# Logits moved into the bank of the turned SoLU row, and the expert picked ahead of the SoLU product

## The chip, the cores and the metric

The kernel runs on one core of one Trainium2 chip. The metric is the device time of one execution in microseconds (us), as the median of several runs. Matrix products run on TensorE, elementwise work and reductions on VectorE, activations and copies on ScalarE, small arithmetic and the scattered stores on GpSimd, and loads are issued by SyncE. A matrix product writes to PSUM, which has eight banks of 512 float32 columns for each of the 128 partitions.

## The reference

Three parts follow one another on 4608 tokens (8 batches of 576) of width 512.

- Attention through packed keys: for each batch and head, 32 pack rows attend to 576 keys and values (`p_packed`), and then the 576 queries attend to these 32 packed rows.
- A SoLU layer: `h = x @ w_in` (width 1024), `solu = h * softmax(h)`, a layer norm over the row with gains `g_ln`, and `ln @ w_out` (back to width 512).
- A mixture of 8 experts: `logits = x @ w_gate`, the expert of a token is the argmax, its weight the softmax probability of that expert, and the output is `gate * (relu(x @ w1[e]) @ w2[e])`.

## The kernel before

The tokens are cut into 36 tiles of 128 tokens, nine for each of four pairs of batches. After a setup, a pipelined loop over the tiles does attention, SoLU and the choice of the expert; each tile's rows are scattered to memory, sorted by expert. Then a second loop does the experts' two products for the sorted tiles. The change touches the first loop alone.

Every engine has a program of its own, written out by hand as a list of operations for one step t of the loop, and the engines meet only in semaphores. An engine executes its list in that order; when one operation waits, all that stands behind it on its engine waits too. Step t works on several tiles at once: scores and softmax of tile t+1, the up product (into the hidden row `h_ps`) and SoLU of tile t, the down product (into `y_ps`), gate logits and pick of tile t-1, and the rank of tile t-2 within its expert.

The loop's steps are of three kinds. Beside the work that every step has, 12 steps (here called **unit steps**, t mod 9 = 1, 3, 5, 7 in the first three pairs) compute the packed attention of one unit (two heads) of the next pair of batches, and 12 steps (**M steps**, t mod 9 = 2, 4, 6, 8 in the first three pairs) fold the packed rows of a unit into `w_in`, to give the matrix M of the next pair. The 12 others are **plain steps** (t = 0, 9, 18 and the nine tiles of the last pair). In three of the M steps (t = 8, 17, 26, **late M steps**) the scores of tile t+1 are computed after `up_hi` and not before it.

The lists of one step, in order, with the operations of unit and M steps in brackets:

- TensorE: `scores(t+1)`, [M: `k_turn_pp`], `rank(t-2)`, `up_hi(t)`, `up_lo(t)`, [unit: `k_scores`], `down_hi(t-1)` chunks 0 to 2 (six products), `logits_t(t-1)`, `down_hi` chunks 3 to 5, [M: `m_half` 0], `turn_logits(t-1)`, `down_hi` chunks 6 and 7, [unit: `k_turn`], `down_lo` 0 to 2, `turn_a(t+1)`, [M: `m_half` 1], [unit: `k_pack`], `down_lo` 3 to 7, `turn_z(t)`.
- VectorE: `max_s(t+1)`, `read_rank(t-2)`, [M: `k_lo`], `z_lo(t-1)`, `max_h(t)`, `sum_s(t+1)`, [unit: `k_max`], `solu(t)`, `row_sum(t)`, [M: `m_lo` 0], [unit: `k_sum`], `pick(t-1)`, `a_lo(t+1)`, [unit: `k_pp`], [M: `m_lo` 1].
- ScalarE: `z_hi(t-1)`, [M: `k_pt`], `exp_s(t+1)`, `z_raw(t-1)`, `exp_h(t)`, `copy_lt(t-1)`, [unit: `k_exp`], [M: `m_hi` 0], `squares(t)`, [unit: `k_et`], `a_hi(t+1)`, `exp_l(t-1)`, [M: `m_hi` 1], `copy_y(t-1)`. In the last pair one copy of expert weights a step (`first_hi`) comes ahead of `copy_y`.
- GpSimd: `factor(t-1)`, `probs(t+1)`, `place(t-2)`, `scatter_y(t-2)`.

Where these show in the profile: `turn_a` and `turn_z` share the helper line L1348 (they differ by what they read, `sbuf` and `hbuf`); `logits_t` is L1455, `turn_logits` L1461, `copy_lt` L732, `down_hi` L1428, `down_lo` L1435, `up_hi` L1407, `m_half` L1306, `m_hi` L650, `m_lo` L915, `k_max` L881, `k_turn` L1272, `k_et` L614 and L616, `k_pack` L1283, `solu` L1001, `squares` L715, `a_hi` L698 (L692 for the tiles of both batches), `z_raw` L727, `z_hi` L721. `pick` is six small VectorE operations, L1025 (reads the turned logits in PSUM) to L1039 (writes `hot`, the expert as a one-hot row). `sum_s` ends with L978. L487 is the first operation of `place`, which adds `hot` of the tile before to `hsum`; the last operation of `pick` waits for it.

Bank 7 holds the turned probabilities (`a_ps`, columns 0 to 255), the logits turned (`LT0`, 256) and turned back (`LG0`, 384), and the ranks (`RK0`, which shares 256). `turn_a(t+1)` writes this bank, so it waits until the first operation of `pick(t-1)` has read it. Banks 2 and 3 hold the turned SoLU row (`t_ps`): `turn_z` writes it, `z_hi` and `z_raw` read it, and then both banks lie idle until the next `turn_z`. The chain of a unit step is `k_scores` (TensorE), `k_max` (VectorE), `k_exp` (ScalarE), `k_turn` (TensorE), `k_et` (ScalarE), `k_pack` (TensorE). That of an M step is `m_half` (TensorE), `m_hi` (ScalarE), `m_lo` (VectorE) for each half; both halves use bank 6, so the second `m_half` waits for the `m_lo` of the first:

```python
                else:
                    pe.wait_ge(m_lo_done, 2 * u + h)
```

Of the kernel before, what the change touches and what calls it, by code (L numbers as in the profile page):

```python
# [17 lines left out]
ACT = mybir.ActivationFunctionType  # L18
AX = mybir.AxisListType

P = 128
B, H, S, DH, NPK = 8, 8, 576, 64, 32
D, F, E = H * DH, 1024, 8
# [21 lines left out]

LT0, LG0 = 2 * P, 3 * P
RK0 = LT0

ET0, KS0 = 2 * P, 512 - (S - 512)

# [1 line left out]
def wait(eng, sem, n):  # L54

    if not isinstance(n, int) or n > 0:
        eng.wait_ge(sem, n)


def moe_kernel(nc, q_t, k_t, v_t, p_t, w_moe, w_exp, g_ln, w_gate, out):  # L60
    y_dram = nc.dram_tensor("y_sorted", [E * CAP, YC], F32, kind="Internal").ap()
    ctx = ExitStack()
    with ctx:
# [55 lines left out]
        ident = sb("ident", [P, P], F32)  # L119
        mask_pp = sb("mask_pp", [P, P], F32)  # L120
        gln = sb("gln", [P, KF], F32)
        wog = sb("wog", [P, KF, NPK], F32)
# [12 lines left out]
        lg = sb("lg", [P, E], F32)  # L135
# [15 lines left out]
        lt = sb("lt", [P, P], F32)  # L151
# [4 lines left out]
        zraw = sb("zraw", [P, F], F32)  # L156
# [40 lines left out]
        a_ps = ps[:, 7, 0:2 * P]  # L197
        x_ps = ps[:, 6, :]
        g_ps = ps[:, 7, :]


        constants_set, zeroed, small_weights_in, numbers_set, numbers_cast, blanks_set = map(
# [66 lines left out]
        def there(t):  # L269
            return 0 <= t < NT  # L270
# [309 lines left out]
        def _(act):  # L580
# [142 lines left out]
            def z_raw(t):  # L723
                act.wait_ge(z_turned, t + 1)
                wait(act, logits_t_done, t)
                wait(act, z_lo_done, t)
                nc.scalar.activation(zraw[:].rearrange("p (a b) -> p a b", a=2), t_ps, ACT.Copy).then_inc(z_raw_done, 1)  # L727

            def copy_lt(t):
                act.wait_ge(logits_t_done, t + 1)  # L730
                wait(act, logits_turned, t)
                nc.scalar.activation(lt[:], g_ps[:, LT0:LT0 + P], ACT.Copy).then_inc(logits_copied, 1)  # L732

            def exp_l(t):
                q = t % 2
# [19 lines left out]
            for t in range(-1, NT + 1):  # L755
                u, v = unit_at(t), m_at(t)
                if there(t - 1):
                    z_hi(t - 1)
                if v is not None:
                    k_pt(v)  # L760
                if there(t + 1):
                    exp_s(t + 1)
                if there(t - 1):
                    z_raw(t - 1)
                if there(t):
                    exp_h(t)
                if there(t - 1):
                    copy_lt(t - 1)
                if u is not None:
                    k_exp(u)  # L770
                if v is not None:
                    m_hi(v, 0)
                if there(t):
                    squares(t)
                if u is not None:
                    k_et(u)
                if there(t + 1):
                    a_hi(t + 1)
                if there(t - 1):
                    exp_l(t - 1)  # L780
                if v is not None:
                    m_hi(v, 1)
                if LAST <= t < LAST + NCH:
                    first_hi(t - LAST)
                if there(t - 1):
                    copy_y(t - 1)
# [49 lines left out]
        def _(dve):  # L836
# [184 lines left out]
            def pick(t):  # L1021

                n = 4 * t
                dve.wait_ge(logits_turned, t + 1)
                nc.vector.tensor_reduce(lg[:], g_ps[:, LG0:LG0 + P].rearrange("p (k e) -> p e k", k=4)[:, 0:E, :],  # L1025
                                        AX.X, ALU.add).then_inc(pick_chain, 1)
                dve.wait_ge(pick_chain, n + 1)
                nc.vector.tensor_reduce(tok[:, 1:2], lg[:], AX.X, ALU.max).then_inc(pick_chain, 1)
                dve.wait_ge(pick_chain, n + 2)
                nc.vector.scalar_tensor_tensor(key[:], lg[:], tok[:, 1:2], rev[:],  # L1030
                                               ALU.is_equal, ALU.mult).then_inc(pick_chain, 1)
                wait(dve, logits_exp, t)
                nc.vector.tensor_scalar(lgs[:], lg[:], tok[:, 1:2], None, ALU.subtract).then_inc(logits_shifted, 1)
                dve.wait_ge(pick_chain, n + 3)
                nc.vector.tensor_reduce(tok[:, 2:3], key[:], AX.X, ALU.max).then_inc(pick_chain, 1)
                dve.wait_ge(pick_chain, n + 4)
                wait(dve, picked_summed, t)
                wait(dve, rank_summed, t)
                nc.vector.tensor_scalar(hot[:], key[:], tok[:, 2:3], None, ALU.is_equal).then_inc(picked, 1)  # L1039
# [10 lines left out]
            for t in range(-1, NT + 2):  # L1050
                u, v = unit_at(t), m_at(t)
                if there(t + 1):
                    max_s(t + 1)
                if there(t - 2):
                    read_rank(t - 2)
                if v is not None:
                    k_lo(v)
                if there(t - 1):
                    z_lo(t - 1)
                if there(t):  # L1060
                    max_h(t)
                if there(t + 1):
                    sum_s(t + 1)
                if u is not None:
                    k_max(u)
                if there(t):
                    solu(t)
                    row_sum(t)
                if v is not None:
                    m_lo(v, 0)  # L1070
                if u is not None:
                    k_sum(u)
                if there(t - 1):
                    pick(t - 1)
                if there(t + 1):
                    a_lo(t + 1)
                if u is not None:
                    k_pp(u)
                if v is not None:
                    m_lo(v, 1)  # L1080
# [128 lines left out]
        def _(pe):  # L1209
# [171 lines left out]
            def turn_a(t):  # L1381
                pe.wait_ge(probs_done, t + 1)
                if t == 0:
                    pe.wait_ge(m_lo_done, 2 * HP)
                if t >= 2:
                    pe.wait_ge(pick_chain, 4 * (t - 2) + 1)
                turn(a_ps, sbuf[:].rearrange("p a b -> p (a b)"), 2, probs_turned)

            def up_parts(t):
# [50 lines left out]
            def turn_z(t):  # L1440
                pe.wait_ge(solu_done, t + 1)
                wait(pe, z_raw_done, t)
                if t == 0:
                    pe.wait_ge(packed_lo, HP)
                    pe.wait_ge(keys_kept, HP)
                turn(t_ps, hbuf, KF, z_turned)

            def logits_t(t):
                pe.wait_ge(z_raw_done, t + 1)
                wait(pe, rank_read, t)  # L1450
                if t == 0:
                    pe.wait_ge(gates_chain, 6)
                for k in range(KF):
                    g = 32 * (k % 4)
                    mm = nc.tensor.matmul(g_ps[g:g + 32, LT0:LT0 + P], wog[:, k, :], zraw[:, k * P:(k + 1) * P],  # L1455
                                          start=(k < 4), stop=(k >= 4))
                mm.then_inc(logits_t_done, 1)

            def turn_logits(t):
                pe.wait_ge(logits_copied, t + 1)  # L1460
                nc.tensor.transpose(g_ps[:, LG0:LG0 + P], lt[:], ident[:]).then_inc(logits_turned, 1)  # L1461

            def rank(t):

# [6 lines left out]
            for t in range(-1, NT + 2):  # L1471
                u, v = unit_at(t), m_at(t)

                late = v is not None and (t + 1) % TPP == 0
                if there(t + 1) and not late:
                    scores(t + 1)
                if v is not None:
                    k_turn_pp(v)
                if there(t - 2):
                    rank(t - 2)  # L1480
                if there(t):
                    up_hi(t)
                if late:
                    scores(t + 1)
                if there(t):
                    up_lo(t)
                if u is not None:
                    k_scores(u, t)
                if there(t - 1):
                    down_hi(t - 1, range(0, 3))  # L1490
                    logits_t(t - 1)
                    down_hi(t - 1, range(3, 6))
                if v is not None:
                    m_half(v, 0)
                if there(t - 1):
                    turn_logits(t - 1)
                    down_hi(t - 1, range(6, KF))
                if u is not None:
                    k_turn(u)
                if there(t - 1):  # L1500
                    down_lo(t - 1, range(0, 3))
                if there(t + 1):
                    turn_a(t + 1)
                if v is not None:
                    m_half(v, 1)
                if u is not None:
                    k_pack(u)
                if there(t - 1):
                    down_lo(t - 1, range(3, KF))
                if there(t):  # L1510
                    turn_z(t)
# [112 lines left out]
```

## Time and profile before

| what | value |
|---|---|
| median of 3 runs | 1098.95 us (1098.42 to 1099.76) |
| the profiled execution | 1097.72 us, of which the span of the trace is 1096.1 us |
| TensorE busy with products | 1012.6 us, 92% of the span |
| VectorE, ScalarE, GpSimd busy | 505.2, 447.8, 284.9 us |
| mean granted TensorE clock | 0.966 of full speed |
| the first loop | from about 78 to 587 us of the span |

A product's record runs from its start to its modelled end, and the next starts before that end; so the distance between starts tells the cost better than the duration. In the timeline neighbouring instructions of one line are merged: the time is that of the first start, the second figure the time they cover, xN how many. A bracket names the idle time ahead of an instruction on its engine and what ended it.

### The profile page before, as it was taken

Reading aid. Unit: us, or ns where it says so; the run is one execution under the profiler, and the core shown is the slowest. Engines: PE = TensorE matmul, PEld = TensorE weight load, DVE = VectorE, ACT = ScalarE, POOL = GpSimd, SP = SyncE. Lnnn points to the kernel's source line nnn. Section 1 sums busy time; section 2 is a strip of 40 time slices with the busy share of each in tenths; the row PEclk is TensorE's granted clock in tenths of the full one; section 3 lists DMA queues with packets and bytes.
Section 4 is the critical chain, followed back from the end, with each engine's and each line's share of the span. In section 5 each row is a group of like instructions: output and inputs, shape, how many; then the busy total and the mean of one; then the engine's idle time right before and its main releaser. Section 6 shows DMA issues by size and latency. Waiting matters only on the chain.

```text
span 1096.1 us, 20129 instructions
## 1 busy us (share of the span) xinstructions
PE 1012.6 (92%) x5707; PEld 795.5 (73%) x5708; DVE 505.2 (46%) x1219; ACT 447.8 (41%) x767; POOL 284.9 (26%) x637
## 2 busy tenths in 40 slices
PE   7548999999999999999994999999999999999994
PEld 4336777777777777777873788888888888888883
DVE  3344666565666656576565252521152431234211
ACT  2344555555555555566552241421241322233110
POOL 1421222222222222245562121221121221222211
PEclk9758999999999999999997999999999999999998
DMA  9301222322122221151103551511152331111110
GB/s 354 108 11 51 67 66 78 97 87 88 58 61 85 87 79 38 37 195 50 39 20 116 193 191 48 190 40 48 38 170 69 114 125 38 46 40 38 48 38 29
DMA packets 64759, 92.62 MB, mean 84 GB/s; under 512 B 42944, under 2 KB 45120, under 8 KB 64704
## 3 DMA queue, kind: packets, MB, share of 16 engines
q1 hardware_dynamic: 55584, 61.96, 17.8%
q0 software_dynamic: 9120, 29.97, 8.0%
q8 instruction: 29, 0.48, 0.2%
q14 instruction: 26, 0.21, 0.1%
HBM read 70.37 MB, written 21.54 MB: 84 GB/s over the span
## 4 chain that ended last, share of the span: by engine, by line
PE 89%; DVE 3%; issue 2%; ACT 2%; DMA 1%; POOL 1%; SPq 0%; ACTq 0%; POOLq 0%; DVEq 0%
PE ps L1341 39%; PE ps L1428 12%; PE ps L1348 8%; PE ps L1407 7%; PE ps L1435 6%; PE ps L1416 3%; PE ps L1377 3%; PE ps L1306 2%; PE ps L1455 2%; PE ps L1263 2%; PE ps L1283 2%; DVE m_odd L915 1%; PE ps L1272 1%; PE ps L1219 1%; POOL w_in L440 1%
## 5 line engine op out<-in xcount | busy, mean ns | idle before, releaser
L1341 PE MATMUL ps<-W,xr 128*128 (+1 forms) x912 | 224.4, 401 | 2.4 <-DVE xr L1084 2.4
L1341 PE MATMUL ps<-W,zr 128*128 x912 | 222.2, 398 | 2.6 <-DVE zr L1157 2.6
L1341 PEld LDWEIGHTS ps<-W,xr 128*128 128x128 f32 x912 | 170.0, 190 | 41.7 <-DVE xr L1084 1.8
L1341 PEld LDWEIGHTS ps<-W,zr 128*128 128x128 f32 x912 | 168.3, 188 | 41.0 <-issue 2.8
L1428 PE MATMUL ps<-w_out,zr 128*128 128x512 f32 x576 | 156.8, 410 | 1.1 <-ACT zr L721 1.1
L1428 PEld LDWEIGHTS ps<-w_out,zr 128*128 128x128 f32 x576 | 101.9, 188 | 39.5 <-issue 16.9
L802 ACT ACTIVATE zr<-ps 128x1024 fp32r<-128x1024 f32 x38 | 39.0, 1025 | 196.6 <-PE ps L1348 196.6
L457 POOL TENSOR_TENSOR small<-half 128x1 f32<-128x1 f32 x77 | 21.6, 280 | 345.1 <-DVE yb L1169 195.4
L461 POOL TENSOR_TENSOR sbuf<-sbuf,msum 128x256 f32<-128x256 f32 x36 | 22.2, 616 | 283.0 <-DVE msum L978 283.0
L797 ACT ACTIVATE hbuf<-ps 128x1024 f32<-128x1024 f32 x38 | 38.8, 1022 | 137.6 <-PE ps L1341 137.6
L1084 DVE TENSOR_TENSOR xr<-ps,xr 128x512 fp32r<-128x512 f32 x39 | 26.9, 691 | 145.6 <-ACT xr L792 145.6
L1169 DVE TENSOR_SCALAR yb<-ps,gate 128x512 f32<-128x512 f32 x38 | 28.5, 751 | 137.7 <-PE ps L1341 137.7
L1435 PE MATMUL ps<-w_out,zr 128*128 128x512 f32 x288 | 81.4, 406 | 0.0
L708 ACT ACTIVATE hbuf<-ps,small 128x1024 f32<-128x1024 f32 x36 | 40.2, 1116 | 99.0 <-DVE small L996 99.0
L1348 PE MATMUL ps<-ident,hbuf 128*128 128x128 f32 x592 | 77.6, 275 | 1.0 <-ACT hbuf L797 0.7
L1348 PEld LDWEIGHTS ps<-ident,hbuf 128*128 128x128 f32 x592 | 69.8, 142 | 11.6 <-ACT hbuf L797 0.9
L1157 DVE TENSOR_TENSOR zr<-ps,zr 128x1024 fp32r<-128x1024 f32 x38 | 46.5, 1225 | 38.5 <-ACT zr L802 38.5
L1019 DVE TENSOR_TENSOR zr<-zraw,zr 128x1024 fp32r<-128x1024 f32 x36 | 44.1, 1225 | 36.4 <-ACT zraw L727 36.4
L1435 PEld LDWEIGHTS ps<-w_out,zr 128*128 128x128 f32 x288 | 51.6, 188 | 11.9 <-issue 2.1
L715 ACT ACTIVATE junk<-hbuf,small 128x1024 bf16<-128x1024 f32 x36 | 41.4, 1149 | 20.6 <-DVE small L1006 20.4
L1001 DVE SCALAR_TENSOR_TENSOR hbuf<-ps,hbuf 128x1024 f32<-128x1024 f32 x36 | 44.0, 1221 | 12.6 <-ACT hbuf L708 12.6
L996 DVE TENSOR_REDUCE small<-ps 128x1 f32<-128x1024 f32 x36 | 43.9, 1219 | 12.8 <-PE ps L1416 12.7
(216 smaller groups left out, 1486.5 us busy)
## 6 DMA issues: line engine op xcount, KB each, us to landing
raw_e<-w_exp SPq DMA_DIRECT2D x48, 512.0 KB, 5.0
qb<-y_sorted POOLq DMA_DIRECT2D x40, 257.0 KB, 3.0
vb<-v_t SPq DMA_DIRECT2D x16, 640.0 KB, 5.6
kb<-k_t SPq DMA_DIRECT2D x16, 576.0 KB, 4.4
qb<-q_t SPq DMA_DIRECT2D x144, 64.0 KB, 3.0
y_sorted<-pad SPq DMA_DIRECT2D x8, 257.0 KB, 4.2
raw_out<-w_moe SPq DMA_DIRECT2D x4, 512.0 KB, 5.0
raw_in<-w_moe SPq DMA_DIRECT2D x4, 512.0 KB, 14.3
```

Source lines behind the costliest of these rows:

```text
L708: nc.scalar.activation(hbuf[:].rearrange("p (a b) -> p a b", a=2), h_ps, ACT.Exp, bias=small[:, 0:1], scale=1.0, accum_out=small[:, 12 + q ...
L715: nc.scalar.activation(junk[:], hbuf[:], ACT.Square, bias=small[:, 16 + q:17 + q], scale=1.0, accum_out=small[:, 4 + q:5 + q]).then_inc(sq ...
L802: nc.scalar.activation(zr[:, 0, :].rearrange("p (a b) -> p a b", a=2), t_ps, ACT.Copy).then_inc(e_hidden_hi, 1)
L996: nc.vector.tensor_reduce(small[:, 0:1], h_ps, AX.XY, ALU.max, negate=True).then_inc(minus_max, 1)
L1001: nc.vector.scalar_tensor_tensor(hbuf[:].rearrange("p (a b) -> p a b", a=2), h_ps, 1.0, hbuf[:].rearrange("p (a b) -> p a b", a=2), ALU.mu ...
L1019: nc.vector.tensor_tensor(zr[:, 1, :], zraw[:], zr[:, 0, :].bitcast(F32), ALU.subtract).then_inc(z_lo_done, 1)
L1157: nc.vector.tensor_tensor(zr[:, 1, :].rearrange("p (a b) -> p a b", a=2), t_ps, zr[:, 0, :].bitcast(F32).rearrange("p (a b) -> p a b", a=2 ...
L1341: mm = nc.tensor.matmul(dst, lhs[:, a, k * P:(k + 1) * P], rhs(b, cols), start=(first and n == 0), stop=(last and n == 2))
L1348: mm = nc.tensor.transpose(dst[:, k * P:(k + 1) * P] if chunks <= 4 else dst[:, k // 4, (k % 4) * P:(k % 4 + 1) * P], src[:, k * P:(k + 1) ...
L1407: nc.tensor.matmul(h_ps[:, h, :], lhs[:, 0, :], M[i % 2][:, part, chunk, h * 512:(h + 1) * 512], start=(n == 0 and part == 0), stop=False)
L1428: nc.tensor.matmul(y_ps, zr[:, 0, k * P:(k + 1) * P], w_out[:, part, k * D:(k + 1) * D], start=(k == 0 and part == 0), stop=False)
L1435: mm = nc.tensor.matmul(y_ps, zr[:, 1, k * P:(k + 1) * P], w_out[:, 0, k * D:(k + 1) * D], start=False, stop=(k == KF - 1))
```

## The change

The logits, turned and turned back, move from bank 7 to bank 2, columns 0 to 255, so `turn_a` no longer waits for `pick`. In its place `turn_z(t)` waits for the first operation of `pick(t-1)`, and `logits_t` drops its wait for the rank. Four operations move: `logits_t` on TensorE ahead of the first six `down_hi` products, `turn_logits` ahead of the second six and of `m_half` 0, `copy_lt` on ScalarE ahead of `exp_h`, and `pick` on VectorE from behind `m_lo` 0 and `k_sum` to directly behind `sum_s`, ahead of `k_max`, `solu` and `m_lo` 0.

```diff
-LT0, LG0 = 2 * P, 3 * P
-RK0 = LT0
+RK0 = 2 * P
+LT0, LG0 = 0, P
...
+        l_ps = ps[:, 2, :]
...
-                nc.scalar.activation(lt[:], g_ps[:, LT0:LT0 + P], ACT.Copy).then_inc(logits_copied, 1)
+                nc.scalar.activation(lt[:], l_ps[:, LT0:LT0 + P], ACT.Copy).then_inc(logits_copied, 1)
...
                     z_raw(t - 1)
+                if there(t - 1):
+                    copy_lt(t - 1)
                 if there(t):
                     exp_h(t)
-                if there(t - 1):
-                    copy_lt(t - 1)
...
-                nc.vector.tensor_reduce(lg[:], g_ps[:, LG0:LG0 + P].rearrange("p (k e) -> p e k", k=4)[:, 0:E, :],
+                nc.vector.tensor_reduce(lg[:], l_ps[:, LG0:LG0 + P].rearrange("p (k e) -> p e k", k=4)[:, 0:E, :],
...
                     sum_s(t + 1)
+                if there(t - 1):
+                    pick(t - 1)
                 if u is not None:
                     k_max(u)
...
                     k_sum(u)
-                if there(t - 1):
-                    pick(t - 1)
                 if there(t + 1):
                     a_lo(t + 1)
...
-                if t >= 2:
-                    pe.wait_ge(pick_chain, 4 * (t - 2) + 1)
+                wait(pe, rank_read, t - 2)
                 turn(a_ps, sbuf[:].rearrange("p a b -> p (a b)"), 2, probs_turned)
...
                 wait(pe, z_raw_done, t)
+                if t >= 1:
+                    pe.wait_ge(pick_chain, 4 * (t - 1) + 1)
...
                 pe.wait_ge(z_raw_done, t + 1)
-                wait(pe, rank_read, t)
...
-                    mm = nc.tensor.matmul(g_ps[g:g + 32, LT0:LT0 + P], wog[:, k, :], zraw[:, k * P:(k + 1) * P],
+                    mm = nc.tensor.matmul(l_ps[g:g + 32, LT0:LT0 + P], wog[:, k, :], zraw[:, k * P:(k + 1) * P],
...
-                nc.tensor.transpose(g_ps[:, LG0:LG0 + P], lt[:], ident[:]).then_inc(logits_turned, 1)
+                nc.tensor.transpose(l_ps[:, LG0:LG0 + P], lt[:], ident[:]).then_inc(logits_turned, 1)
...
                 if there(t - 1):
+                    logits_t(t - 1)
                     down_hi(t - 1, range(0, 3))
-                    logits_t(t - 1)
+                    turn_logits(t - 1)
                     down_hi(t - 1, range(3, 6))
                 if v is not None:
                     m_half(v, 0)
                 if there(t - 1):
-                    turn_logits(t - 1)
                     down_hi(t - 1, range(6, KF))
```

## Rows read from the trace of the kernel before

**Rows 1.** The page's chain of work that ended last, by engine.
```profile
PE 89%; DVE 3%; issue 2%; ACT 2%; DMA 1%; POOL 1%; SPq 0%; ACTq 0%; POOLq 0%; DVEq 0%
```

**Rows 2.** Waits of TensorE, 75 to 600 us: total, times, longest.
```profile
PE ps L1348 <- DVE lg L1025: 16.0, 12, 1.6
...
PE ps L1461 <- ACT lt L732: 2.6, 3, 0.9
```

**Rows 3.** Timeline of an M step: start, duration, engine, line, operation.
```profile
244.55 0.20 DVE L978 RECIPROCAL msum<-msum 128x8 f32<-128x8 f32 x1 [0.26 <-DVE msum L975]
...
245.03 1.22 DVE L1001 SCALAR_TENSOR_TENSOR hbuf<-ps,hbuf 128x1024 f32<-128x1024 f32 x1 [0.28 <-ACT hbuf L708]
...
245.41 0.20 POOL L487 TENSOR_TENSOR hsum<-hsum,hot 128x8 bf16<-128x8 bf16 x1
...
246.50 1.20 ACT L650 ACTIVATE m_even<-ps 64x512 fp32r<-64x512 f32 x2 [1.33 <-PE ps L1306]
...
247.73 1.39 DVE L915 TENSOR_TENSOR m_even<-ps,m_even 64x512 fp32r<-64x512 f32 x2 [1.02 <-ACT m_even L650]
...
249.15 0.19 DVE L1025 TENSOR_REDUCE lg<-ps 128x8 f32<-128x32 f32 x1
...
249.49 0.41 PE L1348 MATMUL ps<-ident,sbuf 128*128 128x128 f32 x2 [1.35 <-DVE lg L1025]
...
249.66 0.95 PE L1306 MATMUL ps<-w_in,pp_r 128*128 128x512 f32 x3
```

**Rows 4.** Timeline of a unit step.
```profile
257.35 1.66 PE L1428 MATMUL ps<-w_out,zr 128*128 128x512 f32 x6
...
258.68 0.72 DVE L881 TENSOR_REDUCE ksm<-ps 128x1 f32<-128x576 f32 x1
...
258.93 0.65 PE L1455 MATMUL ps<-zraw,wog 128*32 128x128 f32 x16
...
260.95 1.15 ACT L715 ACTIVATE junk<-hbuf,small 128x1024 bf16<-128x1024 f32 x1 [0.30 <-DVE small L1006]
...
261.34 0.18 DVE L1025 TENSOR_REDUCE lg<-ps 128x8 f32<-128x32 f32 x1
...
262.21 0.23 DVE L1039 TENSOR_SCALAR hot<-key,tok 128x8 bf16<-128x8 f32 x1
...
262.80 0.60 ACT L614 ACTIVATE eT<-ps 128x512 f32<-128x512 f32 x1 [0.61 <-PE ps L1272]
...
263.62 1.31 PE L1283 MATMUL ps<-vb,eT 128*64 128x128 f32 x20
```

**Rows 5.** Timeline of a plain step and the first product of the next.
```profile
220.41 1.15 ACT L715 ACTIVATE junk<-hbuf,small 128x1024 bf16<-128x1024 f32 x1 [1.32 <-DVE small L1006]
...
221.57 0.38 ACT L698 ACTIVATE aTr<-ps 128x256 fp32r<-128x256 f32 x1
...
224.31 1.88 PE L1407 MATMUL ps<-m_odd,aTr 128*128 128x512 f32 x7
```

**Rows 6.** Timeline of a late M step.
```profile
200.54 1.56 PE L1428 MATMUL ps<-w_out,zr 128*128 128x512 f32 x6
...
202.06 0.65 PE L1455 MATMUL ps<-zraw,wog 128*32 128x128 f32 x16
...
204.14 0.86 PE L1306 MATMUL ps<-w_in,pp_r 128*128 128x512 f32 x3
...
207.27 1.37 DVE L915 TENSOR_TENSOR m_odd<-ps,m_odd 64x512 fp32r<-64x512 f32 x2
```

**Rows 7.** Timeline behind the last tile's `turn_z`.
```profile
579.81 1.02 ACT L727 ACTIVATE zraw<-ps 128x1024 f32<-128x1024 f32 x1
...
579.97 1.67 PE L1428 MATMUL ps<-w_out,zr 128*128 128x512 f32 x6 [1.08 <-ACT zr L721]
```

**Rows 8.** Stretch by stretch: length, PE busy, granted clock (PEclk), DMA.
```profile
104.00:466.00 362.00, 345.43 (x2324) 1.00 0.24 74
```

**Rows 9.** Timeline of step 0: `up_hi` while the clock is low.
```profile
80.46 3.59 PE L1407 MATMUL ps<-m_even,aTr 128*128 128x512 f32 x8
```

## The prediction

> **What bounds the kernel now.** I read the chain of work that ended last, then TensorE's waits, then the timeline of one step of each kind. TensorE carries 89% of the chain [rows 1]: a change is worth what it takes from or adds to TensorE's waits. In the first loop two waits touch this change [rows 2]: 12 times, once in each M step, `turn_a` (L1348) stands for the first operation of `pick` (L1025), 16.0 us in all, 1.33 us each; and in the three late M steps `turn_logits` (L1461) stands 0.9 us for `copy_lt`, 2.6 us in all. At most 18.6 us are to be had.
>
> **What ends the stall in an M step.** In the M step shown [rows 3], VectorE is idle for 1.02 us, starts `m_lo` 0 (L915) at 247.73 when `m_hi` 0 (L650, from 246.50) is done, ends it at 249.12, and starts `pick` at 249.15. `turn_a` starts at 249.49 after 1.35 us of standing, the second `m_half` (L1306) 0.17 us later, at 249.66. But that `m_half` needs the same `m_lo` 0, which ends 0.03 us before `pick` starts. So freeing `turn_a` doesn't free TensorE: it turns the probabilities earlier, and then stands at the second `m_half`.
>
> **The change in an M step.** `pick` now starts behind `sum_s`, whose last operation (L978) ends at 244.75; the turned logits are there by then, because `logits_t` and `turn_logits` each come six products earlier. How long is `pick`? In the unit step, L1025 at 261.34 to L1039 at 262.21 plus 0.23: 1.10 us [rows 4]. So it ends near 245.9, and `solu` starts there, not at 245.03 [rows 3]: 0.85 us late. That eats into VectorE's 1.02 us of idleness ahead of `m_lo` 0, and 0.17 us are left. `m_lo` 0 still starts when `m_hi` 0 is done; `turn_logits` slips in ahead of the first `m_half` but costs next to nothing between products (taken: 0.03 us). `m_lo` 0 then ends at 249.15; from a VectorE end to TensorE takes 0.15 us (L1025 ends at 249.34, `turn_a` starts at 249.49), so the second `m_half` starts at 249.30 instead of 249.66 [rows 3]: **0.36 us gained** of 1.35. Nine ordinary M steps: -3.2 us. Bounds: no gain if the 0.17 us of cover are overrun by 0.36 us; 0.5 us at best (0.34 us from the end of `m_lo` to the start of `turn_a`, plus the 0.17 us of `turn_a` itself).
>
> **Late M steps.** TensorE could begin `down_hi` at 200.54, and `logits_t` ran at 202.06, as soon as `z_raw` was there [rows 6]. With `logits_t` first, TensorE stands 1.52 us from 200.54, and the first `m_half` (204.14) slips by 1.5 us. It took 0.86 us to its end, `m_hi` 0 takes 1.20 us [rows 3], so that ends at about 207.8 and not before; `m_lo` 0, at 207.27 before, starts at about 208.0 (VectorE with `pick`, `solu` and `row_sum` is done at about the same time): +0.7 us, against the 0.36 us that `m_half` gains as above. **+0.33 us** in each of three, +1.0 us; the 0.9 us at `turn_logits` go, but inside this path.
>
> **Unit steps.** Here the moved `pick` has no idle time to fall into. Before, `k_max` (L881) ran at 258.68, directly behind `sum_s`, while `logits_t` had not even begun (258.93) [rows 4]. Now `k_max` stands behind `pick`, and `pick` behind `turn_logits`.
> - `turn_logits` comes ahead by six `down_hi` products, 258.93 - 257.35 = 1.58 us, so `pick` starts at 261.34 - 1.58 = 259.76 and ends 1.10 us later, at 260.86. `k_max` is 2.18 us late.
> - `solu` stands behind `k_max`, and `squares` (L715) behind `solu`: 260.95 + 2.18 = 263.13.
> - `k_et` (L614) stands behind `squares` on ScalarE. From the start of `squares` to that of what follows at once takes 1.16 us (220.41 to 221.57 [rows 5]), so `k_et` starts at 264.29 and not at 262.80. Before, 0.61 us of idleness lay ahead of it; that is used up.
> - `k_pack` (L1283) starts 0.82 us after `k_et` as before: at 265.11 instead of 263.62 [rows 4]. **1.49 us lost.** Part of it shows earlier, at `k_turn`, since `k_exp` is late too; the two are one loss, since `k_pack` bounds behind both.
>
> Twelve unit steps: +17.9 us. Bounds: below, if `k_max` starts as soon as L1039 has started (0.2 us earlier) and the hand-overs are quicker by 0.1 us, 1.2 us each (14.4); above, if `pick` takes 0.2 us more, 1.7 (20.4).
>
> The rule that speaks here is the Trainium skill's (TensorE: Matmul & The Clock Gate, section on the 16 interleaved sub-arrays, where it gives the queues): VectorE's and ScalarE's queues are strictly first in, first out, while TensorE may pull weight loads ahead. The trace agrees as far as it goes: VectorE sat 1.02 us ahead of L915 with `pick` ready behind it [rows 3]. By this rule the sum stands; if `k_max` could pass a waiting `pick`, the unit steps would cost nothing.
>
> **Plain steps.** `solu` is late by at most the whole `pick`, 1.10 us, so `a_hi` (L698) starts at 222.67 at the latest, and `a_lo` follows within about 1 us; `up_hi` at 224.31 needs them [rows 5]. Hidden, as is the new wait of `turn_z`: VectorE does `pick` ahead of `solu`, which `turn_z` needs anyway. `copy_lt` fits while ScalarE waits for `max_h`: nothing. `probs` on GpSimd depends on `sum_s` alone: nothing. SyncE issues nothing here.
>
> **The end of the loop.** Behind the last `turn_z`, six `down_hi` products ran from 579.97 while `z_raw` ran until 580.83 [rows 7]; `logits_t` now waits for it ahead of them: +0.9 us, on the path, since the count of the experts stands behind all products of this step.
>
> **Sum:** -3.2 + 1.0 + 17.9 + 0.9 = **+16.6 us**. The profiled execution goes from 1097.72 us to 1114.3; it lay 1.2 us under the median of the runs shown, so the forecast is 1098.95 + 16.6 = **1115.6 us**.
>
> **Rivals.**
> - *The stall simply goes, and the unit steps don't pay.* For it: [rows 2] name `pick` as the releaser of all 16.0 us, and `turn_a` loses that wait. Then -18.6 us, 1080.4 us. It needs the second `m_half` not to stand, which the 0.03 us between `m_lo` and `pick` speak against. It decides for faster as soon as what M steps gain exceeds what unit steps lose: with 1.33 us gained per M step, from a unit loss under 1.33 us. Chance 0.05.
> - *The stall goes, but the unit steps pay in full:* -18.6 + 17.9 + 0.9 = +0.2 us, 1099.2 us, no change. Same objection for the M steps. Chance 0.03.
> - *Unit steps pay only for `k_max`, about half* (0.75 us, if `k_et` is not bound by `squares`): +7.7 us, 1106.6 us. Chance 0.05.
> - *`pick` delays `m_lo` 0 as well.* Its last operation waits for `hsum` (L487), which ended at 245.61 [rows 3] just before it is wanted, and the cover is 0.17 us. If each M step loses 0.2 us instead of gaining 0.36: +6.7 us on the sum, 1122.3 us. Chance 0.08.
> - *The clock falls.* TensorE gets two short stands in each unit step. At the low level (1.2 GHz) `up_hi` took 3.59 us for its eight products [rows 9], while at full clock seven of them took 1.88 us [rows 5], so eight some 2.1. One such group in each unit step adds 12 x 1.5 = 18 us: 1134 us. Against it: twelve stands of 1.35 us left the granted clock at 1.00 [rows 8], that is 2.4 GHz. The Trainium skill (same page, "A second HAM failure mode: psum-queue depth-cycling") says that frequent short idleness between groups of matmuls can make the clock swing between its levels; no row here shows that. Chance 0.04.
>
> The forecast's own case has 0.75.
>
> **How the numbers follow.** The forecast's case by its bounds runs from 1111 to 1121 us (14.4 and 20.4 for unit steps, -4.5 and 0 for ordinary M steps). To leave out no more than 2 in 10, the range takes in the half-paying case and the delayed `m_lo`: **1106 to 1122.5 us**. Slower by over 0.2% (2.2 us, about what a measurement of this kernel can tell from no change): 0.75 + 0.05 + 0.08 + 0.04 = 0.92; the same 0.03; faster 0.05.
>
> **What would show it.** In the profile after: no wait of `turn_a` for `pick`; twelve waits of the second `m_half` (L1306) for `m_lo` (L915), about 1.1 us each; in unit steps waits of `k_turn` for `k_exp` and of `k_pack` for `k_et`, together about 1.5 us; three waits of `logits_t` for `z_raw`, 1.5 us; VectorE idle ahead of `pick` for about 1 us in unit steps, with TensorE's `turn_logits` as the releaser. The prediction is wrong if `k_et` starts on time in unit steps, if the second `m_half` doesn't stand, or if the granted clock falls under 1.00 between 104 and 466 us.

## The result and the profile after

The changed kernel takes 1115.83 us (median of 4 runs, 1113.25 to 1116.36) against 1098.68 us (4 runs, 1098.12 to 1099.76): ratio 1.015, 95% interval 1.0133 to 1.0168. It is 17 us slower; the forecast was +16.6 us. The profiled execution is the quickest of the four (1113.25 us, span 1111.6), so the traces account for 15.5 us, and the rest is spread between runs.

The chain of work that ended last, which had been TensorE for 89% [rows 1], now goes through VectorE and ScalarE more often:

```profile
PE 82%; DVE 8%; issue 4%; ACT 3%; DMA 1%; POOL 1%; ACTq 0%; SPq 0%; DVEq 0%; POOLq 0%
```

TensorE's waits in the first loop (75 to 620 us; line numbers are one higher than before):

```profile
PE ps L1284 <- ACT eT L617: 8.4, 12, 0.7
PE ps L1307 <- DVE m_odd L916: 8.2, 8, 1.0
PE ps L1273 <- ACT eb L608: 7.5, 12, 0.8
PE ps L1456 <- ACT zraw L728: 6.1, 4, 2.0
PE ps L1307 <- DVE m_even L916: 4.4, 4, 1.3
```

The 16.0 us at `turn_a` and the 2.6 us at `turn_logits` [rows 2] are gone, and so is the 1.1 us for which the first `down_hi` behind the last tile stood for `z_hi` [rows 7]. In their place stand 12 waits of the second `m_half` (L1307) for `m_lo`, 12.6 us in all; 12 waits each of `k_turn` (L1273) and `k_pack` (L1284), 15.9 us, where there were none; and 4 waits of `logits_t` (L1456) for `z_raw`. 19.7 us left, 34.6 us came.

In an M step, the lines that answer to [rows 3]:

```profile
249.76 0.20 DVE L979 RECIPROCAL msum<-msum 128x8 f32<-128x8 f32 x1 [0.26 <-DVE msum L976]
249.88 0.14 DVE L1026 TENSOR_REDUCE lg<-ps 128x8 f32<-128x32 f32 x1
...
251.09 1.22 DVE L1002 SCALAR_TENSOR_TENSOR hbuf<-ps,hbuf 128x1024 f32<-128x1024 f32 x1
...
251.83 1.20 ACT L651 ACTIVATE m_even<-ps 64x512 fp32r<-64x512 f32 x2 [1.62 <-PE ps L1307]
...
253.06 1.39 DVE L916 TENSOR_TENSOR m_even<-ps,m_even 64x512 fp32r<-64x512 f32 x2 [0.30 <-ACT m_even L651]
...
253.20 0.38 PE L1349 MATMUL ps<-ident,sbuf 128*128 128x128 f32 x2
...
254.60 0.94 PE L1307 MATMUL ps<-w_in,pp_r 128*128 128x512 f32 x3 [1.02 <-DVE m_even L916]
```

`pick` runs behind `sum_s` and delays `solu`. `m_lo` 0 still starts when `m_hi` 0 (L651) is done, with 0.30 us of idleness left to VectorE; `turn_a` (L1349) doesn't stand, and the second `m_half` stands 1.02 us.

In a unit step, the lines that answer to [rows 4]:

```profile
262.27 0.65 PE L1456 MATMUL ps<-zraw,wog 128*32 128x128 f32 x16
...
264.35 0.27 PE L1462 MATMUL ps<-ident,lt 128*128 128x128 f32 x1
...
264.66 0.19 DVE L1026 TENSOR_REDUCE lg<-ps 128x8 f32<-128x32 f32 x1 [0.96 <-PE ps L1462]
...
265.70 0.74 DVE L882 TENSOR_REDUCE ksm<-ps 128x1 f32<-128x576 f32 x1
...
267.56 0.77 PE L1273 MATMUL ps<-ident,eb 128*128 128x128 f32 x5 [0.61 <-ACT eb L608]
...
268.00 1.15 ACT L716 ACTIVATE junk<-hbuf,small 128x1024 bf16<-128x1024 f32 x1 [0.50 <-DVE small L1007]
...
269.15 0.57 ACT L615 ACTIVATE eT<-ps 128x512 f32<-128x512 f32 x1
...
269.94 1.31 PE L1284 MATMUL ps<-vb,eT 128*64 128x128 f32 x20 [0.71 <-ACT eT L617]
```

VectorE sits 0.96 us idle for `turn_logits` (L1462) while `k_max` (L882) stands behind `pick`. `k_turn` stands 0.61 us; `k_et` (L615) starts when `squares` (L716) is out of its way, and `k_pack` stands 0.71 us more.

**Where the time went, step by step.** The time from one tile's first `up_hi` product to the next tile's is the length of a step. The columns are the changed kernel (after) and the nine runs of the next section, where each is explained. Each row below is the mean of (length in the kernel named) - (length before) over all steps of the kind, in us; the last row is a single difference.

| | after | pick_back | pick_behind_max | et_first | bank_only | half_early | bank_half | unit_first | logits_behind | pick_ahead_only |
|---|---|---|---|---|---|---|---|---|---|---|
| 12 unit steps | +1.45 | -0.16 | +0.56 | +0.67 | +0.02 | +0.02 | +0.01 | -0.20 | +1.42 | +3.73 |
| 9 M steps | -0.28 | -0.27 | -0.28 | -0.27 | -0.39 | -1.24 | -1.55 | -1.55 | -0.28 | +1.58 |
| 3 late M steps | +0.21 | +0.19 | +0.20 | +0.21 | -0.40 | +0.02 | -0.40 | +0.12 | +0.21 | +2.72 |
| last `up_hi` to the count of the experts | +2.2 | +0.7 | +2.2 | +0.7 | 0.0 | 0.0 | 0.0 | 0.0 | 0.0 | +2.6 |

The plain steps are within 0.05 us of before, except the first (t = 0), in which the clock is still low and which lay from 1.5 us under to 0.95 us over that of before in these traces (after the change: -1.5), and those of the last kernel.

### The profile page after: what moved, and what is told of

Same layout as the page of the kernel before. It is cut to its first block, busy times and chain, and to the rows that moved or that the text cites. A ratio compares the mean times of both kernels' runs of the same rounds, so it can differ in the third digit from the quotient of the medians.

```text
span 1111.6 us, 20093 instructions
## 1 busy us (share of the span) xinstructions
PE 1014.7 (91%) x5707; PEld 798.2 (72%) x5708; DVE 509.3 (46%) x1219; ACT 447.4 (40%) x767; POOL 285.7 (26%) x637
## 4 chain that ended last, share of the span: by engine, by line
PE 82%; DVE 8%; issue 4%; ACT 3%; DMA 1%; POOL 1%; ACTq 0%; SPq 0%; DVEq 0%; POOLq 0%
PE ps L1342 39%; PE ps L1428 9%; PE ps L1349 8%; PE ps L1407 7%; PE ps L1435 5%; PE ps L1416 3%; PE ps L1378 2%; PE ps L1307 2%; PE ps L1264 2%; DVE hbuf L1002 2%; PE ps L1456 2%; PE ps L1284 2%; DVE ksm L882 1%; DVE m_odd L916 1%; POOL w_in L441 1%
## 5 line engine op out<-in xcount | busy, mean ns | idle before, releaser
L1428 PE MATMUL ps<-w_out,zr 128*128 128x512 f32 x576 | 151.2, 410 | 0.0
L1435 PE MATMUL ps<-w_out,zr 128*128 128x512 f32 x288 | 81.4, 406 | 0.0
L1349 PE MATMUL ps<-ident,hbuf 128*128 128x128 f32 x592 | 76.7, 273 | 1.3 <-ACT hbuf L798 0.7
L1349 PEld LDWEIGHTS ps<-ident,hbuf 128*128 128x128 f32 x592 | 69.1, 141 | 11.7 <-ACT hbuf L798 0.9
L716 ACT ACTIVATE junk<-hbuf,small 128x1024 bf16<-128x1024 f32 x36 | 41.4, 1149 | 30.4 <-DVE small L1007 30.1
L1307 PE MATMUL ps<-w_in,pp_r 128*128 128x512 f32 x96 | 31.1, 444 | 22.9 <-POOL w_in L441 10.1
```

The costliest lines, as they stand in the source:

```text
L716: nc.scalar.activation(junk[:], hbuf[:], ACT.Square, bias=small[:, 16 + q:17 + q], scale=1.0, accum_out=small[:, 4 + q:5 + q]).then_inc(sq ...
L1307: mm = nc.tensor.matmul(ps[:, bank, :], pp_r[:, u % 4, a, :], w_in[:, b, c * F + h * 512:c * F + (h + 1) * 512], start=(n == 0), stop=(n = ...
L1349: mm = nc.tensor.transpose(dst[:, k * P:(k + 1) * P] if chunks <= 4 else dst[:, k // 4, (k % 4) * P:(k % 4 + 1) * P], src[:, k * P:(k + 1) ...
L1428: nc.tensor.matmul(y_ps, zr[:, 0, k * P:(k + 1) * P], w_out[:, part, k * D:(k + 1) * D], start=(k == 0 and part == 0), stop=False)
L1435: mm = nc.tensor.matmul(y_ps, zr[:, 1, k * P:(k + 1) * P], w_out[:, 0, k * D:(k + 1) * D], start=False, stop=(k == KF - 1))
```

## The experiments

| kernel | median us | before, same chip | ratio (95% interval) |
|---|---|---|---|
| pick_back | 1096.44 | 1098.32 | 0.9985 (0.997 to 1.0) |
| pick_behind_max | 1105.14 | 1098.32 | 1.0058 (1.0043 to 1.0074) |
| bank_only | 1093.94 | 1098.32 | 0.9963 (0.9949 to 0.9976) |
| half_early | 1087.73 | 1098.32 | 0.9904 (0.9889 to 0.9919) |
| bank_half | 1085.09 | 1099.71 | 0.9867 (0.9849 to 0.9885) |
| logits_behind | 1113.21 | 1099.71 | 1.0129 (1.0102 to 1.0157) |
| pick_ahead_only | 1175.46 | 1099.71 | 1.0674 (1.0648 to 1.07) |
| et_first | 1104.42 | 1098.54 | 1.0055 (1.0039 to 1.0072) |
| unit_first | 1084.69 | 1098.54 | 0.9858 (0.9829 to 0.9887) |

**Only `pick` put back (pick_back).** The edit against the changed kernel:

```diff
                     sum_s(t + 1)
-                if there(t - 1):
-                    pick(t - 1)
...
                     k_sum(u)
+                if there(t - 1):
+                    pick(t - 1)
```

> The changed kernel with pick alone put back behind m_lo 0 and k_sum (banks, waits and all other orders as changed). My theory, that the moved pick in front of k_max and solu is the whole loss of the unit steps: unit steps are back at their old length (1.4 us shorter than in the changed kernel), M steps keep their gain of 0.3 us, late M steps and the end of the loop keep their loss (0.2 us each, and 2.2 us), so about 1099 us (1097 to 1100). Rival, that logits_t and copy_lt ahead of the down products and of exp_h make the loss: the time stays near 1115 us.

Measured 1096.44 us, just under the range; the ratio is 0.9985, with an interval that reaches 1.0: the time of before, or a little less. The waits of `k_turn` and `k_pack` are gone from the trace, those of the second `m_half` and of `logits_t` are as after the change:

```profile
PE ps L1307 <- DVE m_odd L916: 8.2, 8, 1.0
PE ps L1456 <- ACT zraw L728: 6.1, 4, 2.0
PE ps L1307 <- DVE m_even L916: 4.3, 4, 1.3
```

The unit steps fall by 1.6 us each. So the place of `pick` on VectorE is the loss, and `logits_t` ahead is not. They even end 0.16 us shorter than before, which I hadn't expected (unit_first, below).

**`pick` between `k_max` and `solu` (pick_behind_max).** The edit against the changed kernel:

```diff
-                if there(t - 1):
-                    pick(t - 1)
                 if u is not None:
                     k_max(u)
+                if there(t - 1):
+                    pick(t - 1)
                 if there(t):
                     solu(t)
```

> The changed kernel with pick between k_max and solu. My theory, that k_et is bound by squares, which stands behind solu: k_turn no longer waits, solu is 1.36 us late where it was 2.18, and k_pack still stands about 0.7 us in each unit step; 12 x 0.7 = 8.4 us above the kernel with pick put back, so about 1107 us (1105 to 1110). Rival, that the unit steps pay through k_max and k_exp alone: about 1099 us.

Measured 1105.14 us. The wait of `k_turn` is gone and that of `k_pack` remains:

```profile
PE ps L1284 <- ACT eT L617: 8.0, 12, 0.7
```

A unit step still loses 0.56 us with `k_max` on time. So `solu` and `squares`, which have nothing to do with the unit, carry a part of the loss.

**`k_et` ahead of `squares` (et_first).** The other half of the same question; against the changed kernel, on ScalarE:

```diff
+                if u is not None:
+                    k_et(u)
                 if there(t):
                     squares(t)
-                if u is not None:
-                    k_et(u)
```

> The changed kernel with k_et ahead of squares on ScalarE. My theory, that the loss of a unit step is a stand of 0.6 us at k_turn (k_max behind pick) and one of 0.7 us at k_pack (k_et behind squares, which stands behind solu): the stand at k_turn stays, that at k_pack falls to 0.2 us or less; 12 x 0.6 to 0.8 us less than the changed kernel, 1106 to 1109 us. Rival, that k_pack stands for k_exp and k_turn alone: no difference to the changed kernel, 1115 us.

Measured 1104.42 us, somewhat under the range; the unit steps lose 0.67 us and not 1.45. In the waits `k_pack` is no longer found, and `k_turn` stands as in the changed kernel:

```profile
PE ps L1273 <- ACT eb L608: 7.6, 12, 0.8
```

**The bank alone (bank_only).** The new columns, `l_ps` and the three waits of the change, and every order as before.

> The kernel before with the logits in bank 2 and the waits that belong to it, every order as before. My theory, that the second m_half stands for m_lo 0, which pick follows at once: turn_a no longer stands, the second m_half does, about 1.0 us; 12 x 0.3 = 3.6 us faster, 1095 us (1094 to 1097). Rival, that the wait for pick in bank 7 was the stall: 16 us faster, 1083 us.

Measured 0.9963, 4.1 us faster, at the lower edge of the range; the M steps and late M steps gain 0.39 and 0.40 us each, 4.7 us. The wait changed hands:

```profile
PE ps L1307 <- DVE m_odd L916: 7.0, 8, 0.9
PE ps L1307 <- DVE m_even L916: 3.8, 4, 1.2
```

**The first `m_half` earlier, bank 7 kept (half_early).** Against the kernel before:

```diff
                     down_hi(t - 1, range(0, 3))
                     logits_t(t - 1)
-                    down_hi(t - 1, range(3, 6))
                 if v is not None:
                     m_half(v, 0)
                 if there(t - 1):
+                    down_hi(t - 1, range(3, 6))
                     turn_logits(t - 1)
```

> The kernel before, banks and waits unchanged, with the first m_half in front of down_hi 3 to 5, so that m_hi 0 and m_lo 0 can start 1.0 us earlier (then bound by exp_h and row_sum). My theory, that m_lo 0 sets when the M step goes on: turn_a stands about 0.3 us and not 1.33, 12 x 1.0 = 12 us faster, 1087 us (1085 to 1090). Rival, that the bank holds TensorE whatever m_lo does: no change.

Measured 0.9904, 10.6 us faster, with the logits still in bank 7. What is left at `turn_a`:

```profile
PE ps L1348 <- DVE lg L1025: 4.9, 9, 1.2
```

16.0 us in 12 waits [rows 2] became 4.9 in 9. The M steps gain 1.24 us each and the late ones nothing: there `m_hi` 0 stands behind `exp_h` on ScalarE, not behind `m_half`. That is why I overstated the gain with 12 x 1.0.

**Both (bank_half).** The bank, and the first `m_half` earlier.

> Logits in bank 2, pick and all else ordered as before, and the first m_half in front of down_hi 3 to 5. My theory: m_lo 0 ends about 248.1 in the M step shown where TensorE reaches the second m_half at about 248.35, so neither turn_a nor m_half stands; 12 x 1.33 = 16 us faster than before, 1083 us (1081 to 1087). Rival, that VectorE is then bound by solu and row_sum and the stand stays: 1090 us or more.

Measured 0.9867, 14.6 us faster. In the nine M steps neither `turn_a` nor `m_half` stands, and 1.55 us are gained in each; the three late ones still stand for `m_lo`:

```profile
PE ps L1307 <- DVE m_odd L916: 1.5, 2, 0.7
PE ps L1307 <- DVE m_even L916: 0.7, 1, 0.7
```

This is 1.3% below the kernel before, and 31 us below the changed one. An M step gains more here than the 1.33 us of its stand; why is not shown.

**And `logits_t` behind `k_scores` in unit steps (unit_first).** Against bank_half, on TensorE, with `copy_lt` ahead of `exp_h` in unit and late M steps:

```diff
+                first = u is not None
                 if there(t - 1):
+                    if first:
+                        logits_t(t - 1)
                     down_hi(t - 1, range(0, 3))
-                    logits_t(t - 1)
+                    if not first:
+                        logits_t(t - 1)
```

> Logits in bank 2 and the first m_half in front of down_hi 3 to 5, as in the kernel with both, and besides logits_t directly behind k_scores in unit steps alone (copy_lt ahead of exp_h in unit and late M steps), pick where it was before. Unit steps were 0.2 us shorter in the kernel with pick put back than before; if that comes from the place of logits_t behind k_scores, 12 x 0.2 = 2.4 us less than the kernel with both: a ratio to the kernel before of 0.984 to 0.986 and not 0.987, 1082 us. Rival, that it comes from something else: no difference, 0.987.

The unit steps are 0.20 us shorter, as expected, so the place of `logits_t` is the cause. The time doesn't settle it: 0.9858 (0.9829 to 0.9887) against 0.9867, since 2 us are no more than the scatter of these runs. In its trace one late M step of three took 1.5 us longer than the other two, though the second `m_half` stood 1.82 us in each of the three. These are two of the three:

```profile
203.94 0.94 PE L1310 MATMUL ps<-w_in,pp_r 128*128 128x512 f32 x3 [1.82 <-DVE m_odd L919]
...
329.49 1.11 PE L1310 MATMUL ps<-w_in,pp_r 128*128 128x512 f32 x3 [1.82 <-DVE m_even L919]
```

Behind the second the granted clock is 0.60 (329.40 to 333.00 us), and that is the longer step; behind the first and the third it is 1.00. So this trace holds 1.5 us that the lower clock cost, beside what the unit steps gained.

**`logits_t` behind, where it stood for `z_raw` (logits_behind).** In the late M steps and behind the last tile, against the changed kernel:

```diff
+                behind = late or t == NT
                 if there(t - 1):
-                    logits_t(t - 1)
+                    if not behind:
+                        logits_t(t - 1)
                     down_hi(t - 1, range(0, 3))
-                    turn_logits(t - 1)
+                    if behind:
+                        logits_t(t - 1)
+                    else:
+                        turn_logits(t - 1)
                     down_hi(t - 1, range(3, 6))
...
+                    if behind:
+                        turn_logits(t - 1)
                     down_hi(t - 1, range(6, KF))
```

> The changed kernel with logits_t behind the first six down_hi products, and turn_logits behind the second six, in the three late M steps and behind the last tile alone. My theory: the end of the loop gets back its 2.2 us (a stand of 2 us and the lower clock behind it), the late M steps get nothing back, because pick in front of solu then delays m_lo 0 as much; 1113.6 us (1112 to 1115). Rival, that logits_t first costs the late M steps 1.4 us each: 1109.5 us.

Measured 1113.21 us. The late M steps are exactly as long as in the changed kernel (+0.21 us); the stand went to the second `m_half`:

```profile
210.15 0.27 PE L1462 MATMUL ps<-ident,lt 128*128 128x128 f32 x1
...
210.46 0.19 DVE L1026 TENSOR_REDUCE lg<-ps 128x8 f32<-128x32 f32 x1
...
214.71 0.93 PE L1307 MATMUL ps<-w_in,pp_r 128*128 128x512 f32 x3 [2.44 <-DVE m_odd L916]
```

The end of the loop is as long as before.

**`pick` alone ahead (pick_ahead_only).** The kernel before with `pick` moved as in the change and nothing else.

> The kernel before with pick alone moved ahead of k_max, solu and m_lo 0; logits_t, turn_logits and the banks as before, so turn_logits comes 1.5 us later than in the changed kernel and behind the first m_half in M steps. My theory of the queue: each unit step loses 1.5 + 1.58 = 3.1 us, each M step about 1.3 us, together 52 us, about 1151 us (1144 to 1156). Rival, that pick costs only its own 1.1 us wherever it stands: 1098.7 + 12 x 1.1 = 1112 us.

Measured 1175.46 us, ratio 1.0674: 76 us slower, where I had expected 52. The queue does what was expected: `k_turn` stands 2.0 us (24.1 us in 12 waits) and the second `m_half` 2.4. But the lengths are more than that, and the timeline of a unit step shows why:

```profile
292.79 0.77 PE L1272 MATMUL ps<-ident,eb 128*128 128x128 f32 x5 [1.99 <-ACT eb L607]
...
293.31 1.30 PE L1435 MATMUL ps<-w_out,zr 128*128 128x512 f32 x3
...
294.41 0.63 PE L1348 MATMUL ps<-ident,sbuf 128*128 128x128 f32 x2
...
295.18 2.23 PE L1283 MATMUL ps<-vb,eT 128*64 128x128 f32 x20
```

`k_pack` covers 2.23 us and not 1.31 [rows 4]. The stretches behind the stand (length, busy, granted clock, DMA) say it directly:

```profile
291.00:294.00 3.00, 1.21 (x8) 0.95 0.20 74
294.00:297.00 3.00, 2.86 (x22) 0.50 0.00 0
297.00:300.50 3.50, 3.50 (x31) 0.98 0.48 129
```

For 3 us the clock is at 1.2 GHz, half of full. Over the 4.5 us behind a stand the granted clock is 0.62 after nine of the twelve stands of `k_turn` and after six of the twelve of the second `m_half`, and 1.00 after the other nine. The three unit steps in which the clock stayed up lost 2.96 to 2.98 us, near the 3.1 that the queue was expected to cost, and the other nine 3.76 to 4.47; the six M steps in which it stayed up lost 1.00 to 1.16 us, and the other six 2.45 to 2.73. So in these steps the queue cost about what was expected, and the lower clock the rest. Beside them six of the last pair's steps lost 0.80 to 1.65 us each and the end of the loop 2.6 us; no run tells these apart by cause.

My rival "the clock falls" is true of this kernel and not of the changed one's unit steps: after the change the granted clock is 1.00 from 104 to 466 us, as before [rows 8], with its stands of 0.6 and 0.7 us in the unit steps. At the end of its loop the clock did fall (below).

## Why the prediction was right, by its steps

- **"It turns the probabilities earlier, and then stands at the second `m_half`"**: shown. bank_only moved the wait from L1348 to L1306's line and gained 0.39 us a step where 0.36 was forecast; half_early took most of the stall away without touching the bank. The releaser that [rows 2] name, `pick`, was only the next in the queue behind `m_lo` 0.
- **M steps, -3.2 us**: 9 x -0.28 = -2.5 us. bank_only gives the 0.39; the 0.11 us between them is `turn_logits`, now ahead of the first `m_half`. From the first `up_lo` product to the first `m_half` it was 245.55 - 241.04 = 4.51 us before, and 250.87 - 246.25 = 4.62 us after. I had taken 0.03 us for it. The upper bound holds a small misreading: from the end of `m_lo` 0 to the start of `turn_a` are 249.49 - 249.12 = 0.37 us; the 0.34 us counts from the start of `pick`. `pick` fell into VectorE's idle time as forecast (idle ahead of `m_lo` 0 in the step shown: 1.02 us before, 0.30 us after; in the other eight 0.52 to 0.80 us were left).
- **Late M steps, +1.0 us**: 3 x 0.21 = +0.6 us. `logits_t` stood 1.36 us and not 1.52. Either half of the change is enough for this loss: logits_behind takes the stand away, with `pick` still ahead of `solu`, and gets nothing back (+0.21 us); pick_back keeps the stand with `pick` behind, and loses 0.19 us; with neither (bank_only) the step gains 0.40 us.
- **Unit steps, +17.9 us**: +17.3 us. That is 1.49 us forecast and 1.37 to 1.42 measured in ten of the twelve; two are longer (1.75 and 1.61), the 1.75 in the run's first, slow-clocked stretch. The two parts were told apart: `k_max` alone late costs 0.67 us (et_first), `solu` and `squares` alone 0.56 us (pick_behind_max), and without either the step is 0.16 us shorter than before (pick_back). Against pick_back the two parts are 0.83 and 0.72 us, of 1.61 us for both. The 0.1 us by which I overstated it lies ahead of `k_max`: counted from the start of `k_scores` (256.22 before, 261.15 after), `pick` starts 3.51 us behind it where the forecast had 3.54, and `k_max` follows 1.04 us later (265.70 - 264.66), where I had taken 1.10. So `k_max` is 2.09 us late and not 2.18, `k_et` 1.42 and not 1.49, `k_pack` 1.39 and not 1.49. The 0.16 us of pick_back I hadn't seen.
- **Plain steps, nothing**: ten of eleven within 0.03 us.
- **The end of the loop, +0.9 us**: mis-sized in the profiled run, +2.2 us. `logits_t` stood 2.00 us there, where the first `down_hi` had stood 1.08 us before [rows 7], and the clock fell behind it. These are the lines that answer to [rows 7], and the stretches:

```profile
594.71 1.02 PE L1456 MATMUL ps<-zraw,wog 128*32 128x128 f32 x16 [2.00 <-ACT zraw L728]
595.66 2.83 PE L1428 MATMUL ps<-w_out,zr 128*128 128x512 f32 x6
```

```profile
588.00:593.00 5.00, 4.71 (x27) 1.00 0.14 53
594.70:598.30 3.60, 3.59 (x22) 0.53 0.23 78
```

  In pick_back and et_first the same stand of 2.00 us left the clock up, and the end cost 0.7 us; in pick_behind_max the clock fell as here (0.55 from 584.7 to 588.3 us), and it cost 2.2 us. So the wait is worth some 0.7 us and the clock 1.5 more when it falls.
- **The rivals.** "The stall simply goes" and its mate are refuted by the twelve waits at `m_half`; "unit steps pay only for `k_max`" by pick_behind_max; "`pick` delays `m_lo` 0 as well" by the idleness left ahead of it in all nine ordinary M steps. In the late ones VectorE had no idle time there, before or after, and `pick` does delay it (logits_behind). Its cover was thin: in pick_ahead_only, where `turn_logits` comes later, the same `pick` delays it in every M step, and these lose 1.0 us or more with the clock up.

Added up as in the table, the traces give 17.3 - 2.5 + 0.6 + 2.2 = 17.6 us; the first plain step (-1.5 us) and the rest of the program (-0.6 us by the spans) bring it to 15.5. These two lie within what the traces of the other kernels show too: the rest of the program, from the count of the experts on, took 507.7 to 512.3 us in the eleven traces, 508.8 before and 508.2 after. The medians differ by 17.15 us. That the sum of 16.6 us came so close is in part luck: the terms were off by -0.6, +0.7, -0.4 and +1.3 us, which partly cancel, and 1.5 us of the last term hung on whether the clock fell.

## What to carry to other kernels

When a wait is named for one instruction, look at what stands ahead of it in the same queue: if the next consumer needs that earlier one, freeing the named resource only moves the wait down the list (here 0.39 of 1.33 us was gained). Before an operation is moved ahead on an in-order engine, ask in every kind of step what it will wait for there and what stands behind it: `pick` cost nothing where VectorE idled for 1.02 us, and 1.4 us where `k_max` stood behind it. The gain lay at the start of the chain: the producer `m_half` six products earlier gave 10.6 us alone and 14.6 us with the bank.

## What the hardware showed that I had not expected

- Stands of 1.8 to 2.5 us in TensorE can bring the clock down, and often don't. It fell, to 0.50 to 0.62 over the stretches of 3 to 4.5 us that I looked at, behind one of three stands of 1.82 us in unit_first, behind the stand of 2.00 us at the end of the loop in the changed kernel and in pick_behind_max, and behind 15 of 24 stands of 1.98 to 2.50 us in pick_ahead_only. It stayed at 1.00 behind the same 2.00 us in pick_back and et_first, and behind all three stands of 2.44 and 2.45 us in logits_behind:

```profile
104.00:466.00 362.00, 333.72 (x2236) 1.00 0.24 72
466.00:587.00 121.00, 117.24 (x756) 1.00 0.22 73
```

  The shorter ones, 24 of up to 0.8 us and 15 of 1.0 to 1.4 us in the changed kernel and up to 1.6 us before [rows 2], left it at 1.00. So the length of the stand alone doesn't decide; what does is open.
- Six `down_hi` products and `logits_t` behind `k_scores` take less in one order than in the other. From the start of `k_scores` to that of `k_turn` passed 262.06 - 256.22 = 5.84 us before, and 261.66 - 256.01 = 5.65 us in pick_back, where nothing stood either. Before, the weight loads show idle gaps that end in "issue" of 0.81, 0.36 and 0.20 us around them; with `logits_t` directly behind `k_scores` the gap of 0.36 us is no longer there.
